# The sixteenth attention tile ended on its own, TensorE's quiet steps in another order, rounded halves first, and smaller first loads

## Time and profile before

| what | value |
|---|---|
| median of 3 runs | 1221.04 us (1219.96 to 1221.8) |
| profiled execution, its own time | 1223.14 us |
| its span in the trace | 1221.2 us |
| TensorE busy | 1120.3 us (92%) |
| VectorE busy | 930.0 us (76%) |
| ScalarE busy | 701.9 us (57%) |
| POOL busy | 608.5 us (50%) |
| mean granted TensorE clock | 0.961 of full |

### The profile page before, as it was taken

One profiled execution on the slowest core, in us unless ns is written; L12 is line 12 of the kernel. 1 busy time (PEld: TensorE's weight loads), 2 busy tenths in 40 slices (PEclk: granted clock), 3 DMA queues, 4 the chain that ended last, 5 costly groups with the idle time before them and its releaser, 6 DMA issues.

```text
span 1221.2 us, 21057 instructions
## 1 busy us (share of the span) xinstructions
PE 1120.3 (92%) x7360; PEld 1008.9 (83%) x7360; DVE 930.0 (76%) x2088; ACT 701.9 (57%) x1577; POOL 608.5 (50%) x582
## 2 busy tenths in 40 slices
PE   3456998979999999999999989999899999999998
PEld 2334887869889888888987968888789999999998
DVE  7999999979889999899988988969989105300244
ACT  5566777646667765666666665665765524322232
POOL 5666878735446644555545653444745423222221
PEclk9667999979999999999998989999999999999999
DMA  6787997856675687767676656445445667787764
GB/s 223 280 304 255 370 340 292 273 188 210 214 245 208 237 284 276 254 244 247 223 238 206 223 181 220 164 167 189 156 173 196 210 241 258 249 278 255 245 240 147
DMA packets 86504, 287.12 MB, mean 235 GB/s; under 512 B 9600, under 2 KB 13184, under 8 KB 86400
## 3 DMA queue, kind: packets, MB, share of 16 engines
q1 hardware_dynamic: 78912, 270.04, 64.3%
q10 hardware_dynamic: 7488, 15.73, 3.7%
HBM read 247.46 MB, written 38.27 MB: 234 GB/s over the span
## 4 chain that ended last, share of the span: by engine, by line
PE 69%; DVE 18%; POOL 4%; ACT 4%; issue 3%; DMA 0%; ACTq 0%; POOLq 0%
PE ps_f L746 19%; PE ps_f L748 17%; PE ps_f L747 17%; DVE top L971 7%; DVE work L974 6%; PE ps_av L709 6%; DVE part_r L998 3%; PE ps_s L665 3%; PE ps_t L686 2%; PE ps_t L692 2%; PE ps_t L665 1%; DVE drop L980 1%; POOL gate L588 1%; POOL part_o L594 1%; POOL drop L573 1%
## 5 line engine op out<-in xcount | busy, mean ns | idle before, releaser
L746 PE MATMUL ps_f<-gate,w_ring 128*128 128x384 f32 (+2 forms) x896 | 290.5, 324 | 22.5 <-POOL gate L588 20.6
L971 DVE MAX8 top<-work 128x8 f32<-128x576 f32 x432 | 309.1, 742 | 0.1
L746 PE MATMUL ps_f<-xy,w_ring 128*128 128x384 f32 (+2 forms) x896 | 289.7, 323 | 9.1 <-POOL xy L598 6.1
L573 POOL TENSOR_TENSOR drop<-scores,drop 128x576 f32<-128x576 f32 x144 | 207.9, 1444 | 165.7 <-DVE drop L980 165.7
L748 PE MATMUL ps_f<-gate,w_ring 128*128 128x384 f32 (+2 forms) x896 | 282.1, 315 | 0.0
L747 PE MATMUL ps_f<-gate,w_ring 128*128 128x384 f32 (+2 forms) x896 | 282.0, 315 | 0.0
L748 PE MATMUL ps_f<-xy,w_ring 128*128 128x384 f32 (+2 forms) x896 | 280.6, 313 | 0.0
L747 PE MATMUL ps_f<-xy,w_ring 128*128 128x384 f32 (+2 forms) x896 | 280.5, 313 | 0.0
L974 DVE MATCH_REPLACE8 work<-top,work 128x576 f32<-128x576 f32 x288 | 212.7, 738 | 0.0
L746 PEld LDWEIGHTS ps_f<-gate,w_ring 128*128 128x128 f32 x896 | 171.1, 191 | 40.1 <-POOL gate L588 22.2
L746 PEld LDWEIGHTS ps_f<-xy,w_ring 128*128 128x128 f32 x896 | 169.8, 190 | 27.8 <-issue 10.4
(11 more groups left out here) (88 smaller groups left out, 1835.6 us busy)
## 6 DMA issues: line engine op xcount, KB each, us to landing
w_ring<-w_split SPq DMA_DIRECT2D x412, 512.0 KB, 4.1
w_split<-w_ring SPq DMA_DIRECT2D x36, 512.0 KB, 6.3
raw<-wd SPq DMA_DIRECT2D x64, 256.0 KB, 4.9
w_split<-xy SPq DMA_DIRECT2D x28, 512.0 KB, 3.8
kq<-kqd ACTq DMA_DIRECT2D x12, 576.0 KB, 6.2
v_sb<-vd ACTq DMA_DIRECT2D x12, 320.0 KB, 4.0
kq<-kqd SPq DMA_DIRECT2D x4, 576.0 KB, 6.4
out_t<-y_acc ACTq DMA_DIRECT2D x12, 192.0 KB, 3.4
```

The costliest lines, as they stand in the source:

```text
L573: pool.tensor_tensor(slot, scores[:, it.n % S_SLOTS, t - it.first, :], slot, ALU.add).then_inc(masked, 1)
L746: pe.matmul(out, w[:, 0, m], high, start=b == 0, stop=False)
L971: dve.max(top[:, t % T_SLOTS, 8 * r:8 * r + 8], source(t, r)).then_inc(dve_step, 1)
```

## The change

Five things change. (1) The first load is split: k of pair 0 and the first 256 columns of q come first, the rest of q after pair 1; the copy of item 0's scores goes tile by tile in four pieces, and VectorE waits for the first tile alone. (2) In the opening the values product of step s moves behind the scores of step s + 1; the one of step 21 stays. (3) Weight preparations are two a step, steps 5 to 18, and the direct stores are two a step, steps 18 to 21. (4) In VectorE's step for tile 16 the sixteenth tile is ended first, then tile 16's first two rounds follow, then the sum is closed and inverted. (5) The three products of a source run high-high, low weight by high value, then high weight by low value; an opening unit waits for the high half before the first and for the low half before the third. `copy_values` writes the high half before `x_raw`.

The diff, cut to its changed lines with little around them:

```diff
 DIRECT_FROM = 1
-DIRECT_STORE_FROM = 7
 PREP_FROM = DIRECT_FROM + W_SLOTS // 2
+DIRECT_STORE_FROM = 18

...

+FIRST_END = LAST_OF_GROUP[CHUNKS[0].last_gp]
 READY = [values_step(c.last_gp) + 1 for c in CHUNKS]
...

-    s = 5 * (s - PREP_FROM)
-    return range(max(0, s // 3), max(0, min(len(PREP), (s + 5) // 3)))
+    s = 2 * (s - PREP_FROM)
+    return range(max(0, s), max(0, min(len(PREP), s + 2)))
+def stored_pieces(s):
+    s = 2 * (s - DIRECT_STORE_FROM)
+    return range(max(0, s), max(0, min(W_SLOTS, s + 2)))

...
     for it in ITEMS:
+        if it.last == FIRST_END:
+            continue
         if it.last + INV_LAG - starts_early(it.gp) == t:
...

+        kq_first = sem("kq_first")
         kq_loaded = [sem("kq_loaded%d" % p) for p in range(PAIRS)]
...
         x_high_done = sem("x_high_done")
+        x_copied = sem("x_copied")
         x_low_done = sem("x_low_done")
...

-            load_kq(0, 0)
+            sp.dma_start(kq[:, 0, S:2 * S], kqd[0, :, S:2 * S]).then_inc(kq_first, 16)
+            sp.dma_start(kq[:, 0, 0:2 * P], kqd[0, :, 0:2 * P]).then_inc(kq_first, 16)
             load_raw(0)
             load_kq(0, 1)
+            sp.dma_start(kq[:, 0, 2 * P:S], kqd[0, :, 2 * P:S]).then_inc(kq_loaded[0], 16)
             for j in range(1, RAW_SLOTS):
...
                     load_raw(JOB_OF[PREP[i]] + RAW_SLOTS)
-                if 0 <= s - DIRECT_STORE_FROM < W_SLOTS:
-                    store_direct(s - DIRECT_STORE_FROM)
+                for a in stored_pieces(s):
+                    store_direct(a)
                 while g < len(STREAM) and s >= STEP_OF_UNIT[LAST_UNIT_OF_PIECE[g - W_SLOTS]]:
...
             def low_x(gp):
-                pool.wait_ge(x_high_done, gp + 1)
+                pool.wait_ge(x_copied, gp + 1)
                 for high, low, cols in x_parts(gp):
...
             def score(it):
-                if it.rows in (0, 2):
+                if it.n == 0:
+                    pe.wait_ge(kq_first, 32)
+                elif it.rows == 2 or it.rows == 0 and it.gp:
                     pe.wait_ge(kq_loaded[it.pair], 16 * (it.b + 1))
...
                 need(pe, p_t_copied, it.n)
-                need(pe, x_high_done, it.gp)
+                need(pe, x_copied, it.gp)
                 p = probs[:, it.n % P_SLOTS, :]
...
                 pe.wait_ge(p_t_copied, ITEM_OF[LAST_OF_GROUP[gp]].n + 1)
-                need(pe, x_high_done, gp)
+                need(pe, x_copied, gp)
                 for c in range(KC + 1):
...
                     w = w_ring[:, g % W_SLOTS, :, :]
+                    first, end = b == 0, b == u.sources - 1
                     if u.hidden:
-                        if not u.layer and not u.block and u.i == 0:
-                            pe.wait_ge(x_low_done, u.chunk.last_gp - CK + 1 + b + 1)
-                        if u.layer and not u.block and u.i == 0:
-                            pe.wait_ge(y_low_done, Y_OF[u.chunk.n, b].y + 1)
                         high, low, out = x_of(u.chunk, 0, b), x_of(u.chunk, 1, b), as_x(u.chunk, bank(u))
...
                         source = GATE_OF[u.segment, b]
-                        if u.i == 0:
-                            pe.wait_ge(gate_low_done[u.layer], source.in_layer + 1)
                         high, low, out = gate[:, 0, source.slot, 0:u.width], gate[:, 1, source.slot, 0:u.width], bank(u)
-                    end = b == u.sources - 1
-                    pe.matmul(out, w[:, 0, m], high, start=b == 0, stop=False)
-                    pe.matmul(out, w[:, 0, m], low, start=False, stop=False)
-                    mm = pe.matmul(out, w[:, 1, m], high, start=False, stop=end)
+                    opens = u.i == 0 and not (u.hidden and u.block)
+                    gp = u.chunk.last_gp - CK + 1 + b
+                    if opens and u.hidden and not u.layer:
+                        pe.wait_ge(x_high_done, gp + 1)
+                    elif opens and u.hidden:
+                        pe.wait_ge(y_high_done, Y_OF[u.chunk.n, b].y + 1)
+                    elif opens and not u.layer:
+                        pe.wait_ge(read_by_act, source.by_act)
+                    elif opens:
+                        pe.wait_ge(gate_high_done, source.in_layer + 1)
+                    pe.matmul(out, w[:, 0, m], high, start=first, stop=False)
+                    pe.matmul(out, w[:, 1, m], high, start=False, stop=False)
+                    if opens and u.hidden and not u.layer:
+                        pe.wait_ge(x_low_done, gp + 1)
+                    elif opens and u.hidden:
+                        pe.wait_ge(y_low_done, Y_OF[u.chunk.n, b].y + 1)
+                    elif opens:
+                        pe.wait_ge(gate_low_done[u.layer], source.in_layer + 1)
+                    mm = pe.matmul(out, w[:, 0, m], low, start=False, stop=end)
                 if end:
...
                     feed(u)
+                if s - 1 in VALUES_AT and s < READY[0]:
+                    values(VALUES_AT[s - 1])
                 if s == READY[0] - 1:
...
                     transpose(OUT_AT[s])
-                if s in VALUES_AT and s < READY[0]:
+                if s == READY[0] - 1:
                     values(VALUES_AT[s])
...
                 dst = scores[:, it.n % S_SLOTS, :, :]
+                if it.n == 0:
+                    for a in range(2):
+                        for j, src in enumerate(score_halves(it)):
+                            act.wait_ge(scores_done, j + 1)
+                            op = act.activation(dst[:, a, j * PART:(j + 1) * PART], src[:, a, 0:PART], ACT.Copy)
+                        op.then_inc(scores_copied, 1)
+                    return
                 for j, src in enumerate(score_halves(it)):
...
                     act.wait_ge(unit_done, last_hidden2(old[gp // PAIRS % 2 if b == 2 else 1]) + 1)
-                act.activation(x_raw[:, gp % 2, 0:width], ps_av[:, 0:width], ACT.Copy)
                 for high, low, cols in parts:
...
                 op.then_inc(x_high_done, 1)
+                act.activation(x_raw[:, gp % 2, 0:width], ps_av[:, 0:width], ACT.Copy).then_inc(x_copied, 1)
                 if gp // PAIRS % 2 and b + 1 < B:
...

+            def finish_first(t, count):
+                dve.wait_ge(dve_step, count)
+                top8(t - 1, 2)
+                dve.wait_ge(dve_step, count + 1)
+                drop8(t - 1, 2)
+                dve.wait_ge(dve_step, count + 2)
+                top8(t - 1, 3)
+                dve.wait_ge(dve_step, count + 3)
+                find_drop(t - 1)
+                dve.wait_ge(scores_copied, 2 * ITEM_OF[t].n + 2)
+                top8(t, 0)
+                dve.wait_ge(dve_step, count + 4)
+                dve.tensor_scalar(neg_max[:, t % 8:t % 8 + 1], top[:, t % T_SLOTS, 0:1], -SCALE, None,
+                                  ALU.mult).then_inc(neg_max_ready, 1)
+                drop8(t, 0)
+                dve.wait_ge(dve_step, count + 5)
+                top8(t, 1)
+                dve.wait_ge(dve_step, count + 6)
+                drop8(t, 1)
+                close_sum(ITEM_OF[t - 1])
+                dve.wait_ge(dve_step, count + 8)
+                invert_sum(ITEM_OF[t - 1])
...
                 before = count
+                if t == FIRST_END + 1:
+                    finish_first(t, count)
+                    count += 8
+                    continue
                 if new:
                     it = ITEM_OF[t]
-                    if t == it.first:
+                    if t < 2:
+                        dve.wait_ge(scores_copied, t + 1)
+                    elif t == it.first:
                         dve.wait_ge(scores_copied, 2 * it.n + 2)
...
                     last_top = count
-                soon = shut and shut.last == LAST_OF_GROUP[CHUNKS[0].last_gp]
-                if soon:
-                    close_sum(shut)
-                    count += 1
                 if new:
...
                     count += 1
-                if soon:
-                    dve.wait_ge(dve_step, count - 1)
-                    invert_sum(shut)
                 for u in third:
                     event(u)
-                if shut and not soon:
+                if shut:
                     close_sum(shut)
...
                     find_drop(t - 1)
-                if shut and not soon:
+                if shut:
                     dve.wait_ge(dve_step, count)
...
```

## The result

The changed kernel takes 1211.11 us (median of 6 runs, 1210.01 to 1215.92), the kernel before 1221.42 us beside it (6 runs, 1219.96 to 1222.59): a ratio of 0.9921, 95% interval 0.9902 to 0.9939, so 10.3 us faster. The forecast of 1212.5 was 1.4 us off, inside its range. Most of its mechanisms came; two of its steps did not, and two others (the first loads and the values) were worth about twice what they were put at.

A forecast was written before the change was run, and what follows sets the result against it. VectorE's top-32 search paces the opening, VectorE and TensorE are both nearly full from 119 to 213 us, TensorE is full from 258. Terms of -0.6 -2.7 +0.8 +0 -1.5 -0.6 -3.9 = -8.5 from 1221.04 give 1212.5 us, range 1206 to 1219.5.

The forecast's parts named there:

- First loads: Kernel start: smaller first transfer and finer first score copy let VectorE start sooner, -0.6 us (bounds -1.5 to +0.4).
- Values after the next score: Opening steps 10, 14, 18: scores no longer wait behind values, removing two VectorE waits, -2.7 us (bounds -2.7 to 0).
- Two preparations a step: Opening: lighter DMA against a shorter raw-ring cycle, so raw pieces may land late for ScalarE, +0.8 us (bounds 0 to +6).
- Sixteenth tile first: VectorE's steps T16 and T17: 12.0 to 12.8 us against 12.45, so 0.0 (bounds -0.5 to +1.3); TensorE's stream starts earlier.
- The wait at 190.82: VectorE's 1.46 us wait for ScalarE behind TensorE's units goes with TensorE's lead, -1.5 us (0 to -1.5).
- The drop mask at 123.71: VectorE's 1.77 us mask, slowed by POOL's mask, returns to 0.51 once preparations end earlier, -0.6 us (-1.3 to 0).
- Rounded halves first: TensorE's opening units: two products no longer wait for the low half, 3.4 after 258 us plus 0.5 before, -3.9 us.
- the first: Rival: ScalarE stays late, waiting for the values' end instead of scores, and VectorE's stalls stay; 1216.7 us, chance 0.14.
- Drop masks did not collide: Rival: VectorE's drop masks meet POOL operations and wait, four collisions of 1.26, +5.0 us, 1217.5 us; chance 0.10.
- the third rival: The raw ring paces the opening: each pair's second piece lands late, ScalarE late up to 1.8 a pair; 1224.3 us, chance 0.07.
- The fourth: Rival: the clock holds full through the 256 to 260 us stretch and a second such place; 1208.5 us, chance 0.13.
- ScalarE's waits for raw pieces above 16 us: One of the signs named beforehand that would show the prediction wrong; these waits were 15.6 us in the kernel before.

The follow-up runs named there:

- without part 2: Changed kernel with the values products of steps 9, 13 and 17 ahead of the next scores again: 1218.78 us, 0.9974 of the kernel before.
- part 4 undone: Changed kernel with VectorE's old interleaved steps for tiles 16 and 17: 1210.74 us, 0.9912 of the kernel before.
- parts 1, 2 and 5: Changed kernel with old preparations, direct stores and VectorE steps for tiles 16 and 17 restored: 1209.32 us, 0.9901 of the kernel before.
- part 2 alone: Kernel before with only the values product moved after the next score: 1216.74 us, 0.9958 of the kernel before.

## Why the prediction was right, and where it was not

**The number** came out by terms that moved against each other, so that it came within 1.4 us is in good part luck. First loads, values and halves, as found below, make 1.1 + 5.1 + 6.1 = 12.3 us, near the 12.5 of the kernel with these three alone; the whole change gives 10.3, so the other two parts seem to take some back. Forecast and found, in the order of its sum:

- *First loads*, -0.6: 1.14 us at VectorE's first search, 1.8 by its third tile. The transfer was under-sized. Over the kernels of this study the first score started at 4.00 to 4.29 us with the split load and at 4.69 to 5.19 with the whole one, 0.83 us between the means, where 0.3 was taken "since the start-up is shared". Both halves landed 2.8 us after their issue. The Trainium skill, DMA: Bandwidth & Descriptors, section Anatomy of one DMA, gives its figures for transfers that GpSimd issues, while these are SyncE's. By its figures 288 KB would take 2.0 + 0.66 = 2.7 us, an estimate that agrees; for the 576 KB it gives 3.3, against 4.25 in the earlier trace rows, so its price of 0.4 for the split was half of what was measured.
- *Values after the next score*, -2.7: -5.1 alone. VectorE gained by the mechanism put down, but ScalarE's new waits are mostly for raw pieces, which the working had put under the preparations. The size was wrong because the third wait of VectorE, 1.6 us, had been set aside as "part of the tile below"; without the early sum it goes too, and VectorE gained 4.4.
- *Two preparations a step*, +0.8: nothing that the runs can tell. The waits for raw pieces that the working feared did come, but with part 2 (25.9 us with it alone) and not with this part (16.1 us with it and without part 2); and at the sums ahead of the sixteenth tile's VectorE lost only 0.59 and 0.42 us.
- *Sixteenth tile first*, 0.0 on VectorE: this is the step that failed. "Mask 1.4 and exponential 1.0 end at 6.4 to 7.0" took ScalarE to be free when the mask is done. The mask was in time; ScalarE stood at a raw piece, 3.98 us, with the copies of values, a normalising and the partner tile's exponential to follow, and the sum came at T16 + 10.6. That queue had been priced under the preparations, with 0.3 us of room read from a step of the old order; pulling the sum forward took the room away, and the 0.3 no longer held. With it went "3.5 us earlier on top of the -2.5" for the stream: 117.93 instead of 113. The early products added their part: they ran 5.05 us instead of 3.33, at a granted clock of 0.50 from 105 to 109. TensorE had idled 4.35 us up to 101.31; the clock fell just after 100 and came back after 110, while in the kernel before it was back at 108.6, ahead of these products. The old steps give the start that this part was to give, 113.94 with part 4 undone, and it buys no time either.
- *The wait at 190.82*, -1.5: it stayed, 1.47 us, at 189.40, and also in the kernels whose stream started 4 us sooner still (1.46 us at 185.01 in that of parts 1, 2 and 5). It moves along with the stream; the lead that was to swallow it doesn't reach it. *The drop mask at 123.71*, -0.6: 1.77 us there became 1.06, and the 14 drop masks from 119 to 213 us take 10.7 us instead of 12.0. Timeline of the changed kernel:

```profile
125.16 1.06 DVE L1015 TENSOR_SCALAR drop<-scores,top 128x576 f32<-128x576 f32 x1
...
189.40 0.75 DVE L1033 SCALAR_TENSOR_TENSOR part_r<-part_r 128x256 f32<-128x256 f32 x1 [1.47 <-ACT part_o L919]
```

- *Rounded halves first*, -3.9: -6.1 alone. The mechanism was right, and the 3.4 us after 258 came in sum, if not in each opening. What was under-sized is the part before 258, put at 0.5 with the earlier openings "inside VectorE's pace: 0". PE's groups from 100 to 258 us in the changed kernel:

```profile
L766 PE MATMUL ps_f<-xy,w_ring 128*128 128x256 f32 x128 | 38.9, 304 | 2.0 <-ACT scores L846 0.8 <-ACT xy L896 0.5 <-ACT part_o L919 0.4
L774 PE MATMUL ps_f<-xy,w_ring 128*128 128x256 f32 x128 | 37.0, 289 | 0.7 <-POOL xy L592 0.6 <-POOL xy L612 0.2
...
L766 PE MATMUL ps_f<-gate,w_ring 128*128 128x256 f32 x119 | 35.1, 295 | 3.2 <-ACT part_o L919 1.9 <-ACT gate L932 1.3
L774 PE MATMUL ps_f<-gate,w_ring 128*128 128x256 f32 x118 | 34.8, 295 | 6.8 <-POOL gate L602 6.8
```

  12.7 us, where the kernel before has 3.4 + 11.1 = 14.5 in the same stretch, with the same openings: 1.8 less, not 0.5. Some of these openings stand at a granted clock of 0.50 (244 to 248 us in the stretches above), where a product moved under the wait saves more; how much that adds no run separates.

**The rivals.** ScalarE did not stay late for scores (17.5 us to 5.3), which rules out the first. Drop masks did not collide in the opening: up to 119 us only two took over 0.55 us, 0.80 and 0.62. A late raw piece, as in the third rival, did bite, once, for some 2.3 of the 4.29 us at the sixteenth tile; that this cost the forecast so little is shown by the kernels that take the wait away and gain 0 to 2 us. The fourth came in part, and at more than one place. The stretch at 1.2 GHz, which in the kernel before lasts 13.6 us (248.6 to 262.2, from its inside), took 6.8 in the changed kernel's trace (243.5 to 250.3). Behind 130 us the kernel before has four more, 6.8 us each near 214, 658 and 727 us and 3.4 near 882; the changed kernel has none near 210 and 3.4 us at each of the other three. From two of these places, stretches of the kernel before:

```profile
212.00:216.00 4.00, 2.96 (x14) 2.96 (x15) 4.00 (x10) 3.00 (x8) 3.58 (x5) 0.50 0.23 57
724.00:728.00 4.00, 2.37 (x10) 2.24 (x10) 1.81 (x6) 1.90 (x4) 3.81 (x4) 0.50 0.00 0
```

and of the changed kernel:

```profile
208.00:212.00 4.00, 1.81 (x9) 1.21 (x10) 4.00 (x13) 4.00 (x11) 3.07 (x5) 1.00 0.24 90
716.00:720.00 4.00, 2.63 (x15) 2.37 (x16) 3.45 (x9) 1.30 (x3) 1.20 (x1) 0.76 0.59 220
```

Half of TensorE's busy time at 0.50, behind 130 us, is 15.3 us in the kernel before and 6.9 in the changed one: an estimate of what the clock can have given, up to 8.4 of the 12.8 us between the two traced executions. Up to 6.0 of it lies between the marks of 190.97 and 272.60, where the changed kernel gains 5.8 us and the waits above are at most 1.8 less. It is an upper bound, since TensorE does not set the pace everywhere, and the kernel with part 4 undone, at 11.6 by the same estimate, is as fast. How much of the gain is the clock's no run isolates.

**The tests named beforehand.** VectorE's start (6.86, forecast near 7.4) and the copies of the scores came as said, the openings after 258 in their sum and in six of eleven singly. The stream's start did not; and of the two sums of the earlier trace rows that were to have no idle, one keeps 0.42, while a new one at 37.31 idles 0.59. "ScalarE's waits for raw pieces above 16 us" was a bad test: with part 2 alone they were 25.9 us while VectorE waited at no sum. A wait of an engine with time to spare only tells something beside the wait of the one that it feeds.

## What to carry to other kernels

Where an accumulation has terms that don't need the late operand, run these first and put the wait right ahead of the one that does; it is the work under the wait that pays, and the new order with the old wait is worth nothing. Before a step is pulled forward, list what stands ahead of it on every engine that it passes through, with the loads that those wait for: room that was measured in the old order is not there in the new one. A lead of 3 to 5 us won ahead of a stall that comes anyway may be spent there, so undo the parts of a change one by one, and together, before keeping them all.

## What the runs showed of the hardware

The stretch at 1.2 GHz after the stall near 245 us lasted between 6.8 and 13.6 us in the traces of this study, for the products of the same units: 6.8 in the changed kernel, 10.2 in the kernel of parts 1, 2 and 5, 13.6 in the kernel before. None of these edits was aimed at it. With the other such stretches behind 130 us TensorE was at 1.2 GHz for 37.4 us in the kernel before, 17.0 in the changed one and 20.4 to 30.6 in those of its variants that are as fast. Within one kernel the slower runs go with a lower mean granted clock: in that of parts 1, 2 and 5, 1214.38 us at 0.959 and 1207.89 at 0.979; in the changed kernel, 1215.92 at 0.963 and 1210.01 at 0.977. And a 256 KB load took 7.4 us to land when a 576 KB load was issued 0.2 us behind it on another queue, beside stores of 512 KB; the page of the changed kernel gives 4.6 us as the median of all 64 such loads. Which of these neighbours held it no run isolates.
